# Attention, routed experts and a gated convolution block on one core: low parts of one weight matrix move from GpSimd to VectorE

## The reference

```python
logits = np.einsum('bsd,de->bse', x, w_gate)            # 8 experts
local_gate = sigmoid(x @ w_local)
...
fresh_e = int(np.argmax(logits[b, s]))
e = fresh_e if s == 0 or local_gate[b, s] < 0.5 else prev_e
p = softmax(logits[b, s])
h = np.maximum(x[b, s] @ w1[e], 0.0)                    # 512 -> 1024
out[b, s] = p[e] * (h @ w2[e])                          # 1024 -> 512
```

## Time and profile before

| | us |
|---|---|
| median of 3 runs | 779.76 |
| lowest and highest | 779.73, 787.46 |
| profiled execution, its own time | 785.7 |
| its span, first to last instruction | 784.0 |

### The profile page before, as it was taken

One profiled execution on the slowest core, in us unless ns is written; L12 is line 12 of the kernel. 1 busy time (PEld: TensorE's weight loads), 2 busy tenths in 40 slices (PEclk: granted clock), 3 DMA queues, 4 the chain that ended last, 5 costly groups with the idle time before them and its releaser, 6 DMA issues.

```text
span 784.0 us, 14869 instructions
## 1 busy us (share of the span) xinstructions
PE 739.0 (94%) x4838; PEld 614.9 (78%) x4838; DVE 436.3 (56%) x1034; ACT 308.0 (39%) x608; POOL 335.0 (43%) x442
## 2 busy tenths in 40 slices
PE   6999999999839998999999999999599999999998
PEld 4787777777627886888888888887399998989986
DVE  5777878778677433544445444453259746546420
ACT  4777787677420013111111311100058544535521
POOL 7668787887317359554444854400421100000000
PEclk9999999999958999999999999999699999999999
DMA  8888787774143773434343443100321110010011
GB/s 175 204 219 215 185 225 192 212 181 112 36 154 96 236 226 125 141 138 167 136 168 134 146 167 135 66 28 28 97 66 34 51 38 28 14 40 14 28 41 54
DMA packets 99703, 93.11 MB, mean 119 GB/s; under 512 B 62108, under 2 KB 71604, under 8 KB 99636
## 3 DMA queue, kind: packets, MB, share of 16 engines
q1 hardware_dynamic: 80196, 46.27, 21.9%
q10 hardware_dynamic: 15968, 34.67, 12.7%
q0 software_dynamic: 3472, 11.28, 4.9%
HBM read 76.13 MB, written 16.06 MB: 118 GB/s over the span
## 4 chain that ended last, share of the span: by engine, by line
PE 59%; DMA 5%; POOL 3%; DVE 2%; issue 2%; ACT 1%; ACTq 0%; POOLq 0%; SPq 0%; DVEq 0%
PE row_bank L1170 15%; PE wide_bank L1155 14%; PE row_bank L1356 13%; PE wide_bank L1345 12%; DMA x_slots<-x_rows,token_of 5%; POOL ring L870 2%; PE wide_bank L1181 2%; PE bank L1322 1%; PE bank L1136 1%; POOL x_slots L1070 1%; DMA y_tok<-y_sorted,place_i 0%; PE bank L962 0%; DVE x_tr L1377 0%; DMA y_sorted<-y_sb 0%; ACT x_tr L1429 0%
## 5 line engine op out<-in xcount | busy, mean ns | idle before, releaser
L870 POOL TENSOR_TENSOR ring<-raw_w,ring 128x2048 fp32r<-128x2048 f32 x30 | 137.5, 4605 | 87.2 <-ACT ring L860 87.2
L1155 PE MATMUL wide_bank<-ring,xs_tr 128*128 x600 | 146.4, 401 | 6.4 <-POOL ring L870 3.8
L1170 PE MATMUL row_bank<-ring,h_tr 128*128 x600 | 144.9, 397 | 1.9 <-DVE h_tr L1227 1.9
L860 ACT ACTIVATE ring<-raw_w 128x2048 fp32r<-128x2048 f32 x30 | 55.8, 1907 | 226.2 <-DMA raw_w<-in_moe_w_dram 196.6
L1155 PEld LDWEIGHTS wide_bank<-ring,xs_tr 128*128 128x128 f32 x600 | 113.5, 193 | 30.1 <-issue 7.3
L1170 PEld LDWEIGHTS row_bank<-ring,h_tr 128*128 128x128 f32 x600 | 112.0, 190 | 25.2 <-issue 2.1
L1345 PE MATMUL wide_bank<-x_tr,ring 128*128 128x288 f32 x768 | 108.4, 299 | 2.7 <-DVE x_tr L1377 2.7
L1345 PEld LDWEIGHTS wide_bank<-x_tr,ring 128*128 128x128 f32 x768 | 104.3, 190 | 3.9 <-DVE x_tr L1377 3.2
L1356 PE MATMUL row_bank<-ring,g_tr 128*128 128x512 f32 x432 | 100.2, 390 | 1.4 <-DVE g_tr L1384 1.4
L1356 PEld LDWEIGHTS row_bank<-ring,g_tr 128*128 128x128 f32 x432 | 80.4, 188 | 17.7 <-DVE g_tr L1384 1.6
L219 POOL TENSOR_SCALAR bias<-ncum_row,cum_col 128x128 f32<-128x128 f32 (+3 forms) x128 | 67.0, 532 | 48.8 <-DVE row_min L513 37.2
(11 more groups left out here) (191 smaller groups left out, 976.8 us busy)
## 6 DMA issues: line engine op xcount, KB each, us to landing
raw_w<-in_moe_w_dram ACTq DMA_DIRECT2D x12, 2048.0 KB, 9.9
ncum_row<-cum_rows SPq DMA_DIRECT2D x15, 512.0 KB, 4.2
y_sorted<-y_sb SPq DMA_DIRECT2D x25, 256.0 KB
raw_w<-in_moe_w_dram SPq DMA_DIRECT2D x12, 512.0 KB, 4.0
ncum_tail<-cum_rows SPq DMA_DIRECT2D x32, 144.0 KB, 4.4
out_dram<-out_sb ACTq DMA_DIRECT2D x18, 256.0 KB, 2.0
v_nat<-in_v_dram SPq DMA_DIRECT2D x32, 128.0 KB, 2.5
q_nat<-in_q_dram SPq DMA_DIRECT2D x30, 128.0 KB, 4.0
```

The costliest lines, as they stand in the source:

```text
L860: nc.scalar.activation(high, whole, ACT.Copy).then_inc(high_ready, 1)
L870: nc.gpsimd.tensor_tensor(low, whole, high.bitcast(F32), ALU.subtract).then_inc(low_ready, 1)
L1155: last = nc.tensor.matmul(h_bank[:, half, :], xs_tr[:, a, kb, :], ring[:, bass.ds(n, 1), b, at:at + FH].rearrange("p a c -> p (a c)"), sta ...
L1170: last = nc.tensor.matmul(y_bank[:, :], h_tr[:, a, kb, :], ring[:, bass.ds(n, 1), 2 + b, kb * D:(kb + 1) * D].rearrange("p a c -> p (a c)" ...
```

## The change

The low parts of the second expert's w2 (pieces 2 and 3) are computed by VectorE instead of GpSimd. VectorE does it in the first slot, after move_x(0), and counts in a semaphore of its own, `second_low`. GpSimd gathers slots 4 to 7, waits for `second_low` to be 2, and counts both pieces in `low_ready` with a memset of one number; then it goes on with the gathers of slots 8 to 24. `vector_weights` goes from before relu(0) to behind move_h(0).

```diff
     def pool_experts(pool):
-        low_part(pool, 1, 1, 2)
         gather_slots(pool, 4, 8)
-        low_part(pool, 1, 1, 3)
+
+        pool.wait_ge(second_low, PIECES // 2)
+        nc.gpsimd.memset(counted[:, :], 0.0).then_inc(low_ready, PIECES // 2)
         gather_slots(pool, 8, SLOTS)
...
         move_x(0)
-        vector_weights(dve, then)
+        for piece in range(PIECES // 2, PIECES):
+            dve.wait_ge(high_ready, PIECES + piece + 1)
+            whole, high, low = piece_of(1, piece)
+            V.tensor_tensor(low, whole, high.bitcast(F32), ALU.subtract).then_inc(second_low, 1)
         relu(0)
         move_x(1)
         move_h(0)
+        vector_weights(dve, then)
         with dve.Fori(1, SLOTS - 1) as s:
```

More of the change, by code:

```diff
@@ L782, in mixture @@
     free_i = sb("free_i", [1, E], I32)
+    counted = sb("counted", [1, 1])
     WE = KD * F
@@ L827, in mixture @@
     first_loaded = [sem(f"first_loaded{n}") for n in range(6)]
-    high_ready, low_ready = sem("high_ready"), sem("low_ready")
+    high_ready, low_ready, second_low = sem("high_ready"), sem("low_ready"), sem("second_low")
     y_done = sem("y_done")
```

## The result

The changed kernel is faster by 0.62%: over 21 executions of each, the ratio of its time to that of the kernel before is 0.9938, with a 95% interval of 0.9917 to 0.9959. Its median is 779.4 us (778.1 to 783.4). The kernel before had a median of 784.9 us in the same comparison and a far wider spread, 779.2 to 790.5 us. The medians differ by 5.5 us, and 12 of the 21 executions of the kernel before lie above 784 us, none of the changed kernel's. The three executions shown ahead of the prediction (787.5, 779.7, 779.8) were two from the low end and one from the high. The profiled execution of the changed kernel took 782.5 us, span 780.8, against 785.7 and 784.0. Two of the 29 executions of the kernel before that ran beside e1 to e4 took 1236 and 2549 us; no profile shows why, and the ratios leave them out.

What follows compares the result with a forecast made beforehand. TensorE's expert stage was taken as the bound, stalled near 295 us by GpSimd's late low parts: 4.07 us wait plus 1.63 us restart. 779.76 - 5.70 = 774.1 us, other terms costing nothing; range 772.4 to 780.0.

Steps and rivals of the forecast that it cites:

- The mechanism: Expert stage: subtractions on GpSimd delay its gathers, so the third expert's low parts come late and TensorE waits 3.8 us.
- The price of the stall: TensorE near 295 us: 4.07 us late start plus 1.63 us slow restart, 5.70 us to be won.
- The restart: TensorE's slot after the stall runs at the low clock: 13.90 us against 12.27, 1.63 us more.
- The gathers anew: GpSimd's gathers without the two subtractions: last start at 278.6, low parts ready at 288.9.
- cover: Margin before TensorE wants the third expert's low parts at 295.23, with them ready at 288.9: 6.3 us.
- VectorE: First slot: two added subtractions take 4.5 us, end at 240.1 and cost nothing, with 3.1 us of cover.
- the seven operations: Token weights on VectorE, moved behind h_tr: 2.2 us instead of 6.22, ending at 250.5, cost nothing.
- One sign of being wrong: TensorE's second slot: the prediction is wrong if it starts later than 246.16.
- the sum: Whole kernel: 785.7 - 5.7 = 780.0 us for the profiled execution, 779.76 - 5.70 = 774.1 us from the median of three.
- Rival 2: Near 295 us: the usual execution has no such stall, so nothing is won, 779.8 us; chance 0.14.
- The chances: Whole kernel: within 1% 0.91, faster by over 1% 0.06, slower by over 1% 0.03.
- within: Whole kernel: a change of less than 1%, 7.8 us, counted as not told from no change; chance 0.91.

Runs made afterwards that it cites:

- e1: The kernel before with only the token weights moved behind the first slot's h_tr; ratio to the kernel before 1.0011, median 785.7 us.
- e4: The kernel before with four more subtractions of 128x1024 on GpSimd, results unused; ratio to the kernel before 1.0141, median 794.9 us.
- e2: The changed kernel with the token weights back ahead of relu(0), both subtractions on VectorE; ratio to the kernel before 0.9946, median 779.4 us.
- e3: The changed kernel with one of the two subtractions left on GpSimd, behind slot 7's gather; ratio to the kernel before 0.9950, median 779.3 us.
- e5: The kernel before, both subtractions on GpSimd, with four gathers in flight instead of two; ratio to the kernel before 0.9953, median 778.6 us.
- c1: The kernel before without an edit, one more profiled execution; 779.9 us.
- c2: The kernel before without an edit, profiled once more; 782.9 us.
- w3: e5 with w2's filling of unused matmuls in the first slot and last stage; ratio to the kernel before 1.0141, median 794.4 us.
- w2: The changed kernel with TensorE kept busy by unused matmuls of ones, around slot 0 and densely in the last stage; ratio to the kernel before 0.9951, median 778.5 us.
- w5: e5 with only the first slot's filling of unused matmuls (8 and 3); ratio to the kernel before 0.9928, median 779.2 us.

## Why the prediction was right or wrong

**The mechanism: right.** GpSimd's subtractions held up the gathers, the gathers held up the third expert's low parts, and these TensorE. e1 and e2 tell the two parts of the change apart, e3 and e4 move the dose down and up, and e5 removes the wait by another way with the same gain.

**The price of the stall: 5.70 us predicted, 5.46 measured.** The working took the start of slot 4 from the timeline (282.96) and that of slot 6 from the chain (313.20). The timeline has 0.24 us less for slot 6 in the kernel before:

```profile
299.30 7.09 PE L1155 MATMUL wide_bank<-ring,xs_tr 128*128 x24 [3.83 <-POOL ring L870]
...
312.96 1.40 PE L1155 MATMUL wide_bank<-ring,xs_tr 128*128 x5
```

In one view it is 312.96 - 282.96 - 2 x 12.27 = 5.46 us. The restart is 1.39 us of it, not 1.63.

**The gathers anew: right.** Last start 278.6 predicted, 279.70 measured, with the whole stage 0.55 us later; low parts ready at 288.9 and 289.83; cover 6.3 and 6.5 us. Some of this is luck, since two terms were off in opposite ways: up to 268.25 the gathers came every 1.94 us and not every 1.86, and the gap beside the weight load was 4.73 us and not 6.60. The two gathers beside VectorE lost 0.97 us each, between the 0.4 of the earlier trace rows and the 2.3 of a full block. The Trainium skill's rule (SBUF — State Buffer, "Who interferes with whom") has the direction right here, and the measured size is less than half of what it gives.

**VectorE: right.** 4.48 us for 4.5, the seven operations 2.35 us for 2.2, the memset 0.09, just below its 0.1 to 0.3.

**One sign of being wrong came up.** The prediction called itself wrong if the second slot started later than 246.16, and it started at 247.29. VectorE isn't the cause: c1, the kernel before unchanged, has 247.33, and e2, which has the subtractions on VectorE, has 246.12. Slot 0's start and its matmuls at the low clock set it (236.38 and 8.61 us here, 236.38 and 8.62 in c1), and these vary between executions of one kernel. The sign was drawn too narrowly.

**The step that failed** is in the sum: "It ran 5.9 us over the median of the three timed runs, and the sum takes off the same there". For the profiled execution the sum gave 780.0, and the changed kernel's median is 779.4. From the median of three it gave 774.1, 5.3 us too low. That median was no typical execution: over 21 executions the median of before is 784.9. It most likely belonged to those in which the gathers win the race and there is nothing to take off, as in c1 at 779.9; those three timed executions have no trace, so this is argued. From the better base the sum fits, 784.9 - 5.46 = 779.4, but that it fits so closely is partly luck: c1, c2 and e1 had waits of 0, 1.0 and 0 us, and no trace shows that the typical execution has the whole 5.46. Nor is it like for like: the changed kernel's own profiled execution took 782.5, not 780.0. Rival 2 saw that the 5.9 and the 5.7 us might be the same thing, and was right that executions without the stall exist (c1, e1). It was wrong in calling them the usual ones: 7 of the 21 lie at or below 781.1. The argument against it, that the gathers would have to be 4 us quicker with the same loads in the same places, was wrong too: the last gather came 4.3 us sooner in c1 than in the profiled execution (284.78 against 289.09), with the two loads issued 1.2 us later.

**The chances** rested on 1% as what can be told from no change. The interval came out at 0.2% each way, so 0.62% is clear of noise, and "within" with 0.91 said less than the prediction's own 0.73% did. The relative gain that was forecast, 0.73%, lies inside the measured interval, 0.41% to 0.83%.

## What to carry to other kernels

When two timed executions of one kernel differ by as much as a wait in the profile costs, suspect that the wait is there in one and not in the other: measure how far the two sides of the race are apart (here 2.0 us decided), take the saving off the execution that was profiled, and don't carry it to a median of few. Once such a wait is gone, more of the same cure buys nothing: four different edits (two subtractions moved, one moved, gathers four deep, and the whole change) all ended within 1 us of each other. The cure also narrows the spread, here from 11 us to 5.

Take starts that are to be subtracted from one view only; here the chain and the timeline differ by 0.24 us for the same matmuls.

## What was not expected of the hardware

A gather beside a VectorE subtraction of two SBUF inputs took 1.8 to 1.9 us in the changed kernel, e2 and e3, where it takes 0.94 elsewhere; the subtractions took 2.28 us each in all three, with one such gather beside them or two.

A TensorE wait of 0.8 us left the clock full (c2: the slot's matmuls 5.75 us), one of 3.8 us and one of 10.4 us cost 1.4 and 1.75 us of restart. The length of the wait doesn't settle it alone. Ahead of the last slot's output TensorE waits 1.9 us in every profiled execution, and in half of them, 7 of 14, the output's 24 matmuls then took 7.3 to 7.4 us, in the others 5.7 to 5.8. The mean granted clock from 540 to 550 was 0.90 in before and 1.00 in c1. The kernel before shows both lengths, first in the execution of the rows, then in c1:

```profile
547.69 7.31 PE L1170 MATMUL row_bank<-ring,h_tr 128*128 x24 [1.91 <-DVE h_tr L1227]
```

```profile
543.40 5.76 PE L1170 MATMUL row_bank<-ring,h_tr 128*128 x24 [1.91 <-DVE h_tr L1227]
```

Some ten us in which several engines stood still at once (w3), for the most part with no wait that the profile can name, in a kernel whose parts (w2, w5) each run without it.
